# Attention, feed-forward and soft MoE on one core: the softmax sums taken from two running sums by matrix products

## What is computed

```
q_pool = q.reshape(B, H, S // 2, 2, D).mean(axis=3)        # B=4, H=8, S=1152, D=64
scores = scale * (q_pool @ k.T); scores -= max(scores)
attn   = exp(scores); attn = attn / (attn.sum(-1) + 1e-9)
x      = attn @ v                                          # -> 2304 tokens x 512
h      = x @ w_in;  g = where(h > 0, h, exp(min(h, 0)) - 1);  y = g @ w_out      # 512 -> 2048 -> 512
logits = y @ phi;   soft MoE over 32 slots and 8 experts (512 -> 1024 -> 512)
```

## Time and profile before

| what | value |
|---|---|
| median of the runs | 917.2 us |
| the profiled execution's own time | 918.22 us |
| its span, first to last instruction | 916.2 us |
| mean granted TensorE clock | 0.995 of full speed |
| PE busy | 884.3 us (97%) |
| POOL busy | 387.3 us (42%), all before 430 us |

### The profile page before, as it was taken

The page is one execution under the profiler, slowest core; times in us unless marked ns, Lnnn a source line. Parts: engine busy times, 40 slices in busy tenths (PEclk is TensorE's granted clock), DMA queues, the critical chain, the costliest instruction groups (busy, mean ns, idle before and its releaser), DMA issues.

```text
span 916.2 us, 18068 instructions
## 1 busy us (share of the span) xinstructions
PE 884.3 (97%) x7190; PEld 717.6 (78%) x7190; DVE 545.8 (60%) x971; ACT 470.6 (51%) x1017; POOL 387.3 (42%) x269
## 2 busy tenths in 40 slices
PE   4899999999999999998999999999999999999996
PEld 3566666676676666665999999999999999999733
DVE  6878888888888888853664434433433443443423
ACT  3677787877777777686543322322332332322202
POOL 3979999999999999997000000000000000000000
PEclk9999999999999999999999999999999999999998
DMA  7121122222212211303320000200000000476998
GB/s 237 39 75 55 51 79 79 79 79 78 69 63 80 79 50 56 97 1 117 115 69 1 1 1 0 93 1 1 1 1 1 1 1 1 168 244 219 302 369 286
DMA packets 47828, 76.42 MB, mean 83 GB/s; under 512 B 3584, under 2 KB 33408, under 8 KB 47744
## 3 DMA queue, kind: packets, MB, share of 16 engines
q1 hardware_dynamic: 47744, 75.26, 24.5%
HBM read 70.53 MB, written 4.72 MB: 82 GB/s over the span
## 4 chain that ended last, share of the span: by engine, by line
PE 54%; issue 26%; POOL 16%; DVE 2%; ACT 1%; DMA 0%; POOLq 0%; ACTq 0%
POOL acc L1555 11%; PE psum L684 8%; PE psum L686 7%; PE psum L685 7%; PE psum L666 7%; PE psum L668 7%; PE psum L667 7%; POOL acc_early L1555 5%; PE psum L834 2%; PE psum L811 2%; DVE mx L1186 1%; PE psum L620 1%; PE psum L858 1%; PE psum L724 1%; PE psum L704 1%
## 5 line engine op out<-in xcount | busy, mean ns | idle before, releaser
L948 ACT ACTIVATE pt<-psum 128x576 f32<-128x576 f32 x288 | 174.4, 649 | 77.5 <-PE psum L607 77.4
L1186 DVE TENSOR_REDUCE mx<-psum 128x1 f32<-128x512 f32 x256 | 162.4, 678 | 51.4 <-PE psum L570 51.2
L620 PE MATMUL psum<-pt,vs 128*64 128x288 f32 x1152 | 153.6, 412 | 0.0
L1555 POOL TENSOR_TENSOR acc<-acc,pt 128x576 f32<-128x576 f32 x94 | 148.6, 1581 | 0.3 <-ACT pt L948 0.3
L1390 DVE TENSOR_SCALAR gf<-gf 128x384 f32<-128x384 f32 x96 | 34.5, 360 | 190.5 <-ACT gf L1102 190.5
L1102 ACT ACTIVATE gf<-psum 128x384 f32<-128x384 f32 x96 | 47.2, 492 | 196.0 <-PE psum L668 195.4
L684 PE MATMUL psum<-gh,W 128*128 128x384 f32 x384 | 131.9, 344 | 0.0
L685 PE MATMUL psum<-gl,W 128*128 128x384 f32 x384 | 128.5, 335 | 0.0
L686 PE MATMUL psum<-gh,W 128*128 128x384 f32 x384 | 128.5, 335 | 0.0
L666 PE MATMUL psum<-xh,W 128*128 128x384 f32 x384 | 128.4, 334 | 0.0
L668 PE MATMUL psum<-xh,W 128*128 128x384 f32 x384 | 128.3, 334 | 0.0
(11 more groups left out here) (171 smaller groups left out, 2060.0 us busy)
## 6 DMA issues: line engine op xcount, KB each, us to landing
ring<-in_w SPq DMA_DIRECT2D x62, 512.0 KB, 5.9
vs<-in_v SPq DMA_DIRECT2D x16, 576.0 KB, 3.8
kraw<-in_kT SPq DMA_DIRECT2D x15, 576.0 KB, 3.7
qraw<-in_qT SPq DMA_DIRECT2D x15, 576.0 KB, 4.7
out<-ob SPq DMA_DIRECT2D x18, 256.0 KB, 3.6
wst<-in_w_in SPq DMA_DIRECT2D x16, 256.0 KB, 2.7
wst<-in_w_out SPq DMA_DIRECT2D x16, 256.0 KB, 3.2
spare_half<-in_w SPq DMA_DIRECT2D x2, 512.0 KB, 7.5
```

What stands on the lines that cost most here:

```text
L620: ins = mm(psum[64 * s:64 * s + 64, O_BANK, 0:HALF], vs[:, p % NB, s, kt * D:(kt + 1) * D], pt[:, i % NPT, s, :], start=(kt == 0), stop=(k ...
L948: act.activation(pt[:, i % NPT, :, :], t_pair(("T", h, kt))[:, :, 0:HALF], ACT.Exp, scale=SCALE)\
L1186: dve.tensor_reduce(mx[:, b, u // 2, s, u % 2:u % 2 + 1], bank, AX.X, ALU.max).then_inc(s_red, 1)
L1555: pool.tensor_tensor(to, one, other, ALU.add).then_inc(s_acc, 1)
```

## The change

POOL's last addition a = a + b is gone. PE multiplies both running sums by ones, into the same PSUM rows: two sets of four products instead of one. The counts of s_acc are 7 for a head step instead of 8 (ADDS), and the table ADDED_AT stays. The second running sum has two buffers, as the first has: b of head step h is `acc2_early[:, h % 2]`, and `qraw[:, h % 2]` in the last two steps. As the memory of `xl` is now read by PE until the sum of head step 29 is multiplied, `x_lo(0)` moves from head step 30 (after its tile 1) to head step 31 (after its tile 1), and waits for that product instead of for POOL.

```diff
-    acc2_early, = overlay(("acc2_early", [P, 2, HALF], F32))
+    acc2_early, = overlay(("acc2_early", [P, 2, 2, HALF], F32))
...
+    ADDS = KT - 2
     def second_acc(h):
-        return acc2_early[:, :, :] if h < NH - 2 else qraw[:, 0, :].rearrange("p (s n) -> p s n", s=2)
+        return acc2_early[:, h % 2, :, :] if h < NH - 2 else qraw[:, h % 2, :].rearrange("p (s n) -> p s n", s=2)
...
-            pe.wait_ge(s_acc, (KT - 1) * h + by_pool)
-            for n in range(4):
-                queries = slice(n % 2 * QUARTER, (n % 2 + 1) * QUARTER)
-                ins = mm(o[32 * n:32 * n + 32, 0:QUARTER], ones[:, 0:32], acc[:, h % 2, n // 2, queries], start=True,
-                         stop=(by_pool == KT - 1))
+            pe.wait_ge(s_acc, ADDS * h + by_pool - 1)
+            for first in (True, False):
+                added = acc[:, h % 2, :, :] if first else second_acc(h)
+                for n in range(4):
+                    queries = slice(n % 2 * QUARTER, (n % 2 + 1) * QUARTER)
+                    ins = mm(o[32 * n:32 * n + 32, 0:QUARTER], ones[:, 0:32], added[:, n // 2, queries], start=first,
+                             stop=(not first and by_pool == KT - 1))
...
-                act.wait_ge(s_acc, (KT - 1) * (old // KT) + ADDED_AT[old % KT])
+                act.wait_ge(s_acc, ADDS * (old // KT) + ADDED_AT[old % KT])
...
             if c == 0:
-                dve.wait_ge(s_acc, (KT - 1) * (NH - 2))
+                dve.wait_ge(s_Sf, n_f[("SUM", NH - 3)] + 1)
...
-                if h == NH - 2 and kt == 1:
+                if h == NH - 1 and kt == 1:
                     x_lo(0)
...
-            done = (KT - 1) * h
+            done = ADDS * h
...
-            pool.wait_ge(s_acc, done + (LAST_ADDED - 1 if h == NH - 1 else KT - 2))
-            add(a, a, b)
```

## The result

The changed kernel takes 923.27 us in the median of four runs (922.38 to 924.52), against 917.19 us of the kernel before in four runs: ratio 1.0062, 95% interval 1.0050 to 1.0074. Timed again beside the experiments it took 923.93 us against 917.46 us, ratio 1.0073 (1.0060 to 1.0085). The forecast was 923.3 us. That the two agree to 0.03 us is luck: the four runs of the changed kernel alone spread over 2.1 us, and its second median is 0.7 us higher. What the forecast earned is the 6 us.

A forecast was written before the change was run, and what follows sets the result against it. PE's queue was taken to bound the kernel, with POOL awaited only before the last two sums. 7.84 us for added sets - 0.2 absorbed - 1.52 for waits = +6.1, so 923.3 us; 8-in-10 range 921.0 to 926.3.

The forecast's parts named there:

- PE's queue paces the middle: Middle head steps: PE, with short round trips to ACT, sets the pace; removing POOL's addition gains nothing there.
- The price of a set: PE's sum in each head step: a second set of four products costs 0.245 us, 7.84 us over 32 steps.
- The rival with 0.38 us: PE's sum: the second set doesn't join the first and costs its whole length, 927.7 us; chance 0.10.
- estimate of 0.31 us: PE's sum: a set priced by a packing gain of 3.07 instead of 4, 10 us in all, some 925.6 us.
- The 0.2 us that I allowed for absorption: First steps and head step 29: other engines set the pace there and absorb 0.2 us of the added PE time.
- The waits at the end: Sums of head steps 30 and 31: PE's waits for POOL of 0.32 and 1.20 us go, together -1.52 us.
- the worst case: Head step 31: POOL's three remaining additions all take 2.4 us, ending at 427.7, still before PE at 428.49.
- the moved xl: DVE's subtraction for xl, 2.90 us, moved later: cost 0, done about 15 us ahead of the feed-forward.
- The window of 100.27 us: Middle stretch from 200 to 300.27 us, taken as eight head steps of 12.5 us each.
- The signs named in the prediction: Changed profile: eight middle steps take 102.2 us; forecast wrong if a step stays 12.5 us, shortens or becomes 12.9.
- the full price: Middle head step: each added set costs its whole 0.38 us, the step becomes 12.9 us; chance 0.10.
- forecast's own range: Total time 922.3 to 924.6 us, from 0.22 to 0.26 us a set and all to none of 1.5 us.

The follow-up runs named there:

- e2: Changed kernel with only the first running sum multiplied, one set a step and POOL's last addition still gone: 916.89 us, ratio 0.9993 to the kernel before.
- e1: Kernel before, POOL's last addition kept, with the complete running sum multiplied by ones twice on PE: 923.64 us, ratio 1.0076.
- e8: Changed kernel timed once more, nothing altered: 923.93 us, ratio 1.0073 to the kernel before.
- e7: Kernel before with one more POOL addition of 128 x 576, result unused, in each of head steps 0 to 25: 934.24 us, ratio 1.0182.
- e3: Changed kernel with the second running sum multiplied three times, so four sets in each head step: 939.40 us, ratio 1.0240 to the kernel before.
- e6: Kernel before with the change in head steps 30 and 31 alone, x_lo(0) not moved: 915.63 us, ratio 0.9982.
- e5: Changed kernel with loops exchanged, each column group taking first and second running sum in a row: 924.55 us, ratio 1.0082 to the kernel before.

## Why the prediction was right

**PE's queue paces the middle: shown.** With an addition less on POOL the step keeps its length (e2), with a set more on PE it grows by 0.25 us whether POOL is relieved or not (e1, e8). The slack that was read, 2.97 us between POOL's end and PE's start, is confirmed from the other side: one addition more used it up in a few steps and then cost 0.75 us a step (e7), just what 1.4 us less 0.65 us of idle time gives.

**The price of a set: shown.** 0.245 us was read from five sets back to back; measured are 0.249 (changed), 0.252 (e1 and e8) and 0.246 (e3, a third of three sets). The rival with 0.38 us fails in e3's row. The prediction's estimate of 0.31 us from the packing figure of the Trainium skill (TensorE: Matmul & The Clock Gate, Part 3: Packing small matmuls, Measured speedup vs the span model) is not met either. But that estimate took the set's own 0.24 us as the time of one product alone. No run here multiplies one group alone, so how much the packing gains over one product after the other is not shown.

**Nothing hides it: shown for the middle.** PE's waits for ACT are 4.8 us in the stretch before and after. The 0.2 us that I allowed for absorption are not seen in either of the places named: the first steps grow by 0.25 and 0.23 us (12.98 to 13.21, and 17.0 to 17.25 from the sum of step 0 to that of step 1 in the kernels without a slow stretch in it), and the step behind the sum of step 28, 12.78 us before, is 13.02.

**The waits at the end: right, slightly small.** 1.71 us went instead of 1.52 (e6 by itself: 1.20 + two sets of 0.25 = 1.70). By the starts of the sums, the wait before that of step 30 gave 12.95 + 0.25 - 12.78 = 0.42 us and that before the last one 6.58 + 0.25 - 5.56 = 1.27, some 0.1 us more each than stands in brackets; why is not shown. POOL's last additions ran as slow as the worst case had them and slower:

```profile
423.94 2.41 POOL L1559 TENSOR_TENSOR acc<-acc,pt 128x576 f32<-128x576 f32 x1
426.30 2.93 POOL L1559 TENSOR_TENSOR acc<-pt 128x576 f32<-128x576 f32 x1
429.19 2.40 POOL L1559 TENSOR_TENSOR qraw<-pt 128x576 f32<-128x576 f32 x1
431.55 2.41 POOL L1559 TENSOR_TENSOR acc<-acc,pt 128x576 f32<-128x576 f32 x1
```

beside these rows of DVE:

```profile
425.35 2.61 DVE L1259 TENSOR_TENSOR xl<-x,xh 128x1536 fp32r<-128x1536 f32 x1
427.91 4.77 DVE L1252 TENSOR_TENSOR W<-wst,W 128x1024 fp32r<-128x1024 f32 x2
```

POOL ended at 433.96, and PE came at 435.71. That the moved xl costs nothing by way of POOL holds with 1.75 us to spare, not more. xl itself was done at 427.96, 13.9 us ahead of the feed-forward's first product.

**A size that was off:** POOL's waits for ACT were to rise by 1.6 us a step and rose by 17.0 / 8 = 2.1. The sum left out that the additions that stay got faster as well. From 200.0 to 300.8 twelve of the 64 before took 1.9 us or more, and only four of 56 in the changed kernel; each of these stands beside a subtraction of DVE of the same size (klr or qlr, the low parts of the keys and the queries). Eight fewer in eight steps, at 0.5 us each, are 0.5 us a step. Of the groups of POOL's additions the second running sum's first one shows it most (from 200 us, eight steps; busy us and mean ns), before:

```profile
L1555 POOL TENSOR_TENSOR acc_early<-pt 128x576 f32<-128x576 f32 x8 | 13.4, 1674 | 0.0
```

and in the changed kernel:

```profile
L1559 POOL TENSOR_TENSOR acc_early<-pt 128x576 f32<-128x576 f32 x8 | 11.3, 1410 | 1.2 <-ACT pt L952 0.9
```

It is of no account for the time.

**Readings that were off.** The window of 100.27 us is not eight head steps: by the starts of the sums a step is 12.599 us, so eight are 100.8. The signs named in the prediction have the same error. Eight steps of the changed kernel are 102.8 us, not 102.2, and its step of 12.85 us looks like the 12.9 us given for the full price, which from the right base would be 12.98. The forecast's own range of 922.3 to 924.6 does not follow from the terms named for it either; from 0.22 to 0.26 us a set and from all to none of the 1.5 us they give 922.5 to 925.3. The time lies in both. None of this enters the forecast, which goes by the price of a set.

**The sum.** 7.84 - 0.2 - 1.52 = 6.1 against 32 x 0.249 - 1.71 = 6.26 in the profiled executions: the allowance of 0.2 us that was not needed and the 0.13 us that the sets cost more add 0.33 us, and the 0.19 us that the waits gave more take off a part of it. So the forecast was 0.14 us too small. The difference of the two spans, 6.2 us, holds besides what the first 60 us differ by from execution to execution (+1.08 us at the first sum and -1.07 behind it, which cancel here by chance).

## What to carry to other kernels

Work taken from an engine that the chain of waits names is worth only what somebody waits for it: look up the deadline (who reads the result, when it was ready, when it was read) in a head step of the middle and at the end separately, for they can have different answers, as here. Work given to the engine that is busy without a gap costs its full length in each round, so a trade between the two belongs only where the wait is: in two steps of 32 it gained 1.8 us (1.2 of them at the place itself), in all of them it lost 6. The price of one more of a kind is best read from a place in the same kernel where several of them stand in a row.

## What the runs showed of the hardware

- Four float32 products of 144 columns, each into its own 32 output columns, take 0.245 us as a set back to back, 0.246 to 0.252 as one more in a head step, and it makes nearly no difference (0.02 us a step) whether the program has them set by set or group by group (e5).
- In the busy time by slices of 10 us, each of the ten profiled executions has one slice up to 430 us with a granted clock of 0.83: 50 to 60 us in the kernel before, 30 to 40 us in the changed one and six others, 410 to 420 in e1 and 400 to 410 in e2. Everywhere else the clock is full until the last 20 us. In finer slices of these four it is half the clock, 1.2 GHz, for some 3 us. In each of the four PE had waited just ahead of it: 1.07 us until 50.39 in the kernel before, 1.39 until 31.81 in the changed one, 1.25 until 412.77 in e1 and until 405.43 in e2. The same waits stand in the other profiles with the clock full behind them, so a wait of that length does not by itself bring the slow stretch. It cost 1.59 us in e2, 1.57 in e1 (14.59 us for a step of 13.02) and 1.1 between the sums of steps 0 and 1 in the kernel before. Part of the spread of 1 to 2 us between runs may come from this, which was not tested, and a difference of that size between two kernels is better read from their steps than from their medians.
- POOL's addition of 128 x 576 takes 1.4 us for the most part, 1.9 us beside DVE's subtractions of 128 x 576 (klr, qlr), and 1.9 to 2.9 us beside those for W and xl, which have two inputs in SBUF too (the rows above). In the kernels before and changed every addition above 1.5 us overlaps one of these; some 30 others in each overlap one and stay at 1.4 us. By this the trace agrees with the Trainium skill (GPSIMD Engine Reference, 1. Specifications), which has POOL's SBUF interfaces shared with DVE and names contention with DVE instructions that have two SBUF inputs.
